# Outputs of an attention pair made beside the next pair's scores

## The chip, the cores and the metric

The kernel runs on one core of one Trainium2 chip, in one launch. The metric is the time of an execution in microseconds (us), as the median of three executions. The core has a matmul engine (TensorE, PE in the profile, with its weight loads listed apart as PEld), VectorE (DVE), ScalarE (ACT), GpSimd (POOL) and SyncE (SP), which issues nearly all transfers.

## The reference

There are 4 sequences of 768 tokens with 8 heads of 48. A gated linear attention comes first, then two feed-forward layers on 3072 tokens of 384 features with 2048 hidden ones, the first with a squared ReLU, the second with SiLU.

```python
for t in range(S):
    state = alpha[:, :, t, :, None] * state + np.einsum('bhd,bhe->bhde', k[:, :, t], v[:, :, t])
    y[:, :, t] = np.einsum('bhd,bhde->bhe', q[:, :, t], state)
x = y as (tokens, 384)
x = relu(x @ w_in) ** 2 @ w_out
g = x @ w2_in;  out = (g / (1 + exp(-g))) @ w2_out
```

## The kernel before

The 768 positions are six units of 128, and a unit holds those positions of all four sequences, 512 tokens. The attention of a unit is done in four pairs of heads, so there are 24 pairs n = 0 to 23 (PAIRS = 4). The first feed-forward layer of unit u runs in 16 steps, F = 16u to 16u + 15, one for each block of 128 hidden features. In step F TensorE makes `first_product` F (nine 128x512 matmuls, L1132: each product is a sum of three, of high and low parts of the operands), then `second_product` F - 2 (nine more, L1146). ScalarE makes three passes on the result of the first (`step` and `square_g`: L1429, L1432, L1435), VectorE one (`low_g`, L1810). The two banks `h_ps` take the first products in turn, by the parity of F; `z_ps` holds the second products' sums.

The attention of pairs 4 to 23 is done beside these steps, while the unit before is in the feed-forward layer. `stage_step` is a table of numbers written out by hand: it says in which step each job of a pair is done, and `beside(F)` gives the jobs of step F. For pairs 9 to 23 the jobs are: A (decays: transpose and two rows of scans on VectorE, L1660, L1688, L1703) in step 4n - 20 or 4n - 21; KQ (keys and queries scaled by the decays, VectorE, L1721, L1735) in 4n - 19; S (scores, TensorE, 64 small matmuls, L1007 and L1018) and I (the state's increment, TensorE, 32 small matmuls, L1040) in 4n - 18; Y (outputs, 64 small matmuls, L1109 and L1117) in 4n - 16. Pair 8 has S and I in step 16, Y in step 17. On TensorE S and Y stand between the first and the second product of their step, I behind the second product. I call such a group of small matmuls between large ones a visit.

The small matmuls write three banks, `jobs`. Scores and turned keys of a pair lie in `job_ps[1]` and `job_ps[2]`; its outputs lie in `job_ps[2]` and `job_ps[0]`. So the scores of pair n wait until the outputs of pair n - 1 have been read:

```python
                if n > PAIRS:
                    wait(pe, y_copied, y_count(n))
```

The reading is done in two parts. ScalarE copies the within-half part into `y_sb` (`y_copy`, L1377), then VectorE adds the other part to it (`y_stage`, L1790) and raises `y_copied`. VectorE also masks the scores (`s_stage`, L1747), and ScalarE copies the turned keys (`kt_copy`, L1366) when they are masked. After `y_copied` SP moves the outputs into `x_raw` (L639) and loads the values of pair n + 2 (L593). Everything on every engine is in program order, with semaphores between the engines. After step 95 the second layer follows (L1175, L1211, L1231), with no attention in it.

Of the kernel before, what the change touches and what calls it, by code (L numbers as in the profile page):

```python
# [6 lines left out]
ALU = mybir.AluOpType  # L7
ACT = mybir.ActivationFunctionType


BATCH, HEADS, SEQ, HD = 4, 8, 768, 48
# [6 lines left out]
UT = BATCH * P  # L18
PAIRS = HEADS // 2
ROWS = 64 + HD  # L20
# [5 lines left out]
HALF = P // 2  # L26
# [125 lines left out]
    return 256 * units if units < UNITS else 256 * (units - 1) + LAST_OUT  # L152


def stage_step(kind, n):

    if n < 2 * PAIRS:
        return {"A": 1, "KQ": 2 if n == PAIRS else 3, "S": 4, "I": 4, "Y": 5}[kind] + 3 * (n - PAIRS)
    if n == 2 * PAIRS:
        return {"A": 13, "KQ": 14, "S": 16, "I": 16, "Y": 17}[kind]  # L160
    return {"A": -20 if n == 2 * PAIRS + 1 else -21, "KQ": -19, "S": -18, "I": -18, "Y": -16}[kind] + 4 * n
# [36 lines left out]
def y_count(n):  # L198

    return min(n, MOVED) if n < PAIRS else n - PAIRS + MOVED  # L200
# [7 lines left out]
def beside(step):  # L208

    jobs = BESIDE.get(step, []) if isinstance(step, int) and step >= 0 else []  # L210
    return sorted(jobs, key=lambda j: ("S", "I", "A", "Y", "KQ").index(j[0]))


def repack_pieces(place):
# [24 lines left out]
def wait(eng, sem, value):  # L239
    if isinstance(value, int) and value <= 0:  # L240
        return
    eng.wait_ge(sem, value)
# [14 lines left out]
def build(nc, q, k, v, alpha, w1_in, w1_out, w2_in, w2_out, out):  # L257
    z_dram = nc.dram_tensor("z_scratch", (UNITS, DM, UT), F32, kind="Internal").ap()
    ctx = ExitStack()
    with ctx:  # L260
# [18 lines left out]
        with ExitStack() as one:  # L279
# [6 lines left out]
            y_sb = [sb(f"y_sb{i}", [ROWS, UT], F32, one) for i in range(2)]  # L286
# [134 lines left out]
        h_ps = [bank(f"h_ps{i}") for i in range(2)]  # L421
        z_ps = [bank(f"z_ps{i}") for i in range(KD)]

        jobs = ctx.enter_context(nc.psum_tensor("jobs", [P, 3 * 512], F32))
        s_ps, y_ps = jobs[:, 0:1024], jobs[:, 512:1536]
        job_ps = [jobs[:, 1024:1536], jobs[:, 0:512], jobs[:, 512:1024]]
# [13 lines left out]
        def v_tile(n):  # L440
            return v_wide[n - MOVED][:, :, 0::2, :] if MOVED <= n < PAIRS else v_sb[n % 2][:]
# [10 lines left out]

        first_y, middle_y, later_y = z_ps[1], z_ps[0], (job_ps[2], job_ps[0])
        half_i = (job_ps[2], job_ps[1])

        half_score = [x[:].rearrange("s b t -> s (b t)")[:, 0:BATCH * HALF] for x in score]
# [12 lines left out]
        kt_copied, y_copied = sem("kt_copied"), sem("y_copied")  # L471
# [470 lines left out]
        def _(pe):  # L942
# [37 lines left out]
            def s_stage(n):  # L980

                wait(pe, k_scaled, n + 1)
                wait(pe, q_scaled, n + 1)

                wait(pe, s_copied, 2 * min(n, PAIRS - 1))
                if n > PAIRS:
                    wait(pe, y_copied, y_count(n))
                if n > PAIRS and has_state(n - 1):
                    wait(pe, state_made, n - PAIRS)
                if n >= PAIRS:  # L990
                    s_halves(n)
                    return
                for b in range(BATCH):
                    for h in (0, 1):
                        r = head_rows(h)
                        last = nc.tensor.matmul(job_ps[1 + h][:, tile(b)], kp[n % 2][r, tile(b)], qp[n % 2][r, tile(b)],
                                                start=True, stop=True)
                last.then_inc(s_made, 1)
# [93 lines left out]
            def y_halves(n):  # L1092

                wait(pe, decayed, n - PAIRS + 1)

                wait(pe, i_copied, PAIRS)
                v_flat = v_tile(n).rearrange("t b h d -> t (b h d)")  # L1100

                def to(bank, b, place):
                    rows = slice(0, 64) if b < 2 else head_rows(1)
                    return later_y[bank][rows, place * HALF:(place + 1) * HALF], 64 if b < 2 else HD
                for half in (0, 1):
                    for b in (0, 2, 1, 3):
                        for h in (0, 1):
                            out_cols, cols = to(h, b, 2 * (b % 2) + half)
                            nc.tensor.matmul(out_cols, half_state[half][head_rows(h), b * HD:b * HD + cols],  # L1109
                                             qp[n % 2][head_rows(h), b * P + half * HALF:b * P + (half + 1) * HALF],  # L1110
                                             start=True, stop=True, skip_group_check=True)
                for h in (0, 1):
                    for b in (0, 2, 1, 3):
                        for half in (0, 1):
                            tokens, at = slice(half * HALF, (half + 1) * HALF), (2 * b + h) * HD
                            out_cols, cols = to(half, b, BATCH + 2 * h + b % 2)
                            last = nc.tensor.matmul(out_cols, v_flat[tokens, at:at + cols],  # L1117
                                                    half_score[h][tokens, b * HALF:(b + 1) * HALF],
                                                    start=True, stop=True, skip_group_check=True)
                last.then_inc(y_made, 1)  # L1120
# [5 lines left out]
            def first_product(u, par, f, w_hi, w_lo, tiles=TILES):  # L1126
                wait(pe, act_made, NF * u + f - 1)
                for kk in tiles:
                    if f == 0:
                        wait(pe, x_lo_made, KD * u + TILES.index(kk) + 1)  # L1130
                    for n, (w, x) in enumerate(((w_hi, x_hi), (w_hi, x_lo), (w_lo, x_hi))):
                        last = nc.tensor.matmul(h_ps[f % 2][:], w[:, f, tile(kk)], x[par][:, kk, :],  # L1132
                                                start=(kk == TILES[0] and n == 0), stop=(kk == TILES[-1] and n == 2))
                if tiles[-1] == TILES[-1]:
                    last.then_inc(h_made, 1)
# [111 lines left out]
            for F in range(STEPS):  # L1247
                u, f = divmod(F, NF)
                if u == 0:
                    wait(pe, w_lo_made, 2 * f + 1)  # L1250
                first_product(u, u % 2, f, win_hi, win_lo, TILES[-1:] if F < 2 else TILES)
                if F == 0:
                    i_stage(PAIRS - 1)
                for kind, n in beside(F):
                    if not behind(kind, n):
                        stage(kind, n)
                if F == LAST_U + 4:
                    pe.wait_ge(held_made, 2)
                    pe.wait_ge(y_copied, y_count(LASTP + 1))
                    nc.tensor.matmul(job_ps[0][0:1, 0:1], all_held[:], ones[:], start=True, stop=True).then_inc(held_summed, 1)  # L1260
                if F >= LAG:
                    u, f = divmod(F - LAG, NF)
                    if u == 0:
                        wait(pe, w_lo_made, 2 * f + 2)
                    second_product(u, f, g_pair(F - LAG), wout_hi, wout_lo, u, 0)
                for kind, n in beside(F):
                    if behind(kind, n):
                        stage(kind, n)
# [69 lines left out]
        def _(act):  # L1338
# [31 lines left out]
            def y_copy(n):  # L1370
                y_slot_free(n // PAIRS, n % PAIRS)
                wait(act, y_made, n + 1)
                if n < PAIRS:
                    nc.scalar.activation(y_sb[n % 2][:], first_y[0:ROWS, :], ACT.Copy).then_inc(y_copied, 1)
                    return

                nc.scalar.activation(y_sb[n % 2][:].rearrange("p (c k t) -> p k c t", c=BATCH, k=2),  # L1377
                                     y_ps[0:ROWS, :].rearrange("p (k x) -> p k x", k=2)[:, :, UT // 2:].rearrange(
                                         "p k (c t) -> p k c t", c=BATCH), ACT.Copy).then_inc(within_copied, 1)
# [276 lines left out]
        def _(dve):  # L1656
# [129 lines left out]
            def y_stage(n):  # L1786

                wait(dve, within_copied, n - PAIRS + 1)
                sums = y_sb[n % 2][:].rearrange("p (h x) -> p h x", h=2)
                nc.vector.tensor_tensor(sums, y_ps[0:ROWS, :].rearrange("p (h x) -> p h x", h=2)[:, :, 0:UT // 2], sums,  # L1790
                                        ALU.add).then_inc(y_copied, 1)
# [94 lines left out]
            for F in range(STEPS):  # L1886
                u, f = divmod(F, NF)
                jobs_here = beside(F)
                for kind, n in jobs_here:
                    if kind == "S":  # L1890
                        s_stage(n)
                    if kind == "KQ":
                        k_stage(n)
                        if n != 2 * PAIRS:
                            q_turn(n)
                            q_stage(n)
# [21 lines left out]
                        a_scan(n)  # L1918
                        a_grow(n)
                for kind, n in jobs_here:  # L1920
                    if kind == "Y" and n != 2 * PAIRS - 1:
                        y_stage(n)
                if F in T_STEP:
                    low_t(T_STEP[F])
# [142 lines left out]
```

## Time and profile before

| | |
|---|---|
| median of 3 runs | 881.98 us (881.14 to 882.66) |
| the profiled execution's own time | 877.95 us |
| its span | 876.3 us |
| PE busy | 862.5 us |
| DVE busy | 541.2 us |
| ACT busy | 437.0 us |
| POOL busy | 104.2 us |
| TensorE clock granted | 1.00 over the span |

The span is the part of an execution that the profile covers. The own time is that of the same execution as the runs' times measure it. Busy times count each engine's own instructions, so an engine that is busy nearly all the span is likely to set it.

### The profile page before, as it was taken

The page shows a single profiled execution, that of the slowest core. Times are in us where ns is not written, and L with a number is a line of the kernel's source. Part 1 is how long each engine was busy: PE and PEld are TensorE (multiplying, and loading weights), DVE is VectorE, ACT ScalarE, POOL GpSimd, SP SyncE. Part 2 cuts the span into 40 slices and gives each one's busy share as a digit, 9 for nine tenths or more (in the row PEclk, how much of TensorE's full clock was granted, in tenths as well). Part 3 has the DMA queues.
Part 4 walks back from the last instruction along what each step waited for, and adds up shares of the span by engine and source line. Part 5 has one row for each costly group of instructions (what it writes and reads, how often), then busy time and mean ns, then how long its engine had stood idle before and what let it go on. Part 6 is the DMA issues. An engine that isn't in the chain of part 4 may idle for free.

```text
span 876.3 us, 17615 instructions
## 1 busy us (share of the span) xinstructions
PE 862.5 (98%) x6834; PEld 707.5 (81%) x6834; DVE 541.2 (62%) x1072; ACT 437.0 (50%) x770; POOL 104.2 (12%) x127
## 2 busy tenths in 40 slices
PE   6999989999999999999999999999999999999998
PEld 6777768788878788788888888888888888888898
DVE  7788876777767667664334556556754446766620
ACT  5765544455446445544666744445434436554510
POOL 3453300000000000000354003003030003000000
PEclk9999999999999999999999999999999999999999
DMA  8885434333333332300412352000130000110010
GB/s 171 229 236 126 99 67 120 74 76 103 71 81 87 102 79 67 103 20 13 149 43 71 61 113 78 0 1 1 46 100 0 1 1 1 36 37 1 1 48 28
DMA packets 134203, 60.03 MB, mean 69 GB/s; under 512 B 81824, under 2 KB 129312, under 8 KB 134112
## 3 DMA queue, kind: packets, MB, share of 16 engines
q1 hardware_dynamic: 130800, 58.14, 26.9%
q8 instruction: 56, 0.92, 0.4%
q10 hardware_dynamic: 3312, 0.69, 0.4%
q14 instruction: 35, 0.29, 0.1%
HBM read 45.02 MB, written 9.44 MB: 62 GB/s over the span
## 4 chain that ended last, share of the span: by engine, by line
PE 93%; DVE 4%; issue 1%; ACT 1%; DMA 0%; DVEq 0%; ACTq 0%
PE z_ps L1146 21%; PE h_ps L1132 21%; PE h_ps L1175 20%; PE z_ps L1211 11%; PE jobs L1211 7%; PE jobs L1231 3%; PE jobs L1007 1%; PE jobs L1040 1%; PE jobs L1109 1%; DVE decay L1703 1%; PE jobs L1018 1%; PE jobs L1117 1%; PE h_ps L1231 1%; DVE decay L1688 1%; PE z_ps L1078 0%
## 5 line engine op out<-in xcount | busy, mean ns | idle before, releaser
L1429 ACT ACTIVATE g<-h_ps 128x512 f32<-128x512 f32 x96 | 57.4, 598 | 177.5 <-PE h_ps L1132 175.4
L1523 ACT ACTIVATE sum<-sum 128x512 f32<-128x512 f32 x96 | 60.6, 631 | 137.2 <-DVE sum L1871 111.9
L1810 DVE TENSOR_TENSOR g_lo<-g,g_hi 128x512 fp32r<-128x512 f32 x96 | 67.6, 705 | 85.4 <-ACT g L1435 85.3
L1871 DVE TENSOR_TENSOR sum<-h_ps,sum 128x512 f32<-128x512 f32 x120 | 83.0, 691 | 57.1 <-PE h_ps L1175 54.4
L1132 PE MATMUL h_ps<-x_hi,win_hi 128*128 128x512 f32 x288 | 115.0, 399 | 1.2 <-ACT g L1429 0.8
L1146 PE MATMUL z_ps<-g_hi,wout_hi 128*128 128x512 f32 x282 | 114.4, 406 | 0.0
L1132 PE MATMUL h_ps<-x_hi,win_lo 128*128 128x512 f32 x288 | 112.4, 390 | 0.0
L1132 PE MATMUL h_ps<-x_lo,win_hi 128*128 128x512 f32 x288 | 112.2, 389 | 0.0
L1146 PE MATMUL z_ps<-g_hi,wout_lo 128*128 128x512 f32 x282 | 110.2, 391 | 0.0
L1146 PE MATMUL z_ps<-g_lo,wout_hi 128*128 128x512 f32 x282 | 110.1, 390 | 0.0
L1175 PE MATMUL h_ps<-s_hi,t_hi 128*128 128x512 f32 x264 | 103.0, 390 | 0.2 <-DVE sum L1871 0.2
L1175 PE MATMUL h_ps<-s_hi,t_lo 128*128 128x512 f32 x264 | 102.7, 389 | 0.0
L1175 PE MATMUL h_ps<-s_lo,t_hi 128*128 128x512 f32 x264 | 102.7, 389 | 0.0
L1866 DVE TENSOR_TENSOR ring_lo<-sum,ring_hi 128x512 fp32r<-128x512 f32 x80 | 58.2, 728 | 64.3 <-ACT ring_hi L1536 64.3
L1132 PEld LDWEIGHTS h_ps<-x_hi,win_hi 128*128 128x128 f32 x288 | 54.0, 188 | 13.8 <-POOL win_lo L835 1.2
L1132 PEld LDWEIGHTS h_ps<-x_hi,win_lo 128*128 128x128 f32 x288 | 54.0, 188 | 11.7
L1146 PEld LDWEIGHTS z_ps<-g_hi,wout_hi 128*128 128x128 f32 x282 | 52.9, 188 | 12.2
L1132 PEld LDWEIGHTS h_ps<-x_lo,win_hi 128*128 128x128 f32 x288 | 54.1, 188 | 10.5
L1432 ACT ACTIVATE g_hi<-g 128x512 fp32r<-128x512 f32 x96 | 60.7, 632 | 3.1
L1146 PEld LDWEIGHTS z_ps<-g_hi,wout_lo 128*128 128x128 f32 x282 | 52.9, 188 | 11.5
L1146 PEld LDWEIGHTS z_ps<-g_lo,wout_hi 128*128 128x128 f32 x282 | 53.0, 188 | 10.0
L1435 ACT ACTIVATE g<-g 128x512 f32<-128x512 f32 x96 | 59.3, 617 | 0.0
(169 smaller groups left out, 1532.8 us busy)
## 6 DMA issues: line engine op xcount, KB each, us to landing
z_scratch<-z_sb SPq DMA_DIRECT2D x18, 256.0 KB, 2.7
pre<-z_scratch SPq DMA_DIRECT2D x18, 256.0 KB, 3.9
v_sb<-in_v SPq DMA_DIRECT2D x44, 96.0 KB, 2.6
out_x<-z_stage SPq DMA_DIRECT2D x80, 48.0 KB, 1.7
nat_a<-in_alpha SPq DMA_DIRECT2D x40, 88.0 KB, 2.3
nat_k<-in_k SPq DMA_DIRECT2D x40, 88.0 KB, 2.4
nat_q<-in_q SPq DMA_DIRECT2D x40, 88.0 KB, 2.2
nat_a<-in_alpha SPq DMA_DIRECT2D x40, 80.0 KB, 2.8
```

Source lines behind the costliest of these rows:

```text
L1132: last = nc.tensor.matmul(h_ps[f % 2][:], w[:, f, tile(kk)], x[par][:, kk, :], start=(kk == TILES[0] and n == 0), stop=(kk == TILES[-1] an ...
L1146: last = nc.tensor.matmul(z_ps[m][:], w[:, f, tile(m)], x, start=(f == 0 and n == 0), stop=(f == NF - 1 and n == 2), skip_group_check=True)
L1175: last = nc.tensor.matmul(bank[:], w[j][:, tile(t)], y[:, x, :], start=(c == 0 and k == 0), stop=(c == len(FACTORS[r]) - 1 and k == 2))
L1211: last = nc.tensor.matmul(pair_bank(t, m), w[f][:, tile(m)], x, start=(first and c == 0), stop=(final and c == 2), skip_group_check=True)
L1231: last = nc.tensor.matmul(token_ps[b][:, 0:DM], x[:, tile(b)], w[f][:], start=(f == 0 and n == 0), stop=(f == NF - 1 and n == 2))
L1429: nc.scalar.activation(g[f % 2][:], h_ps[f % 2][:], ACT.Relu).then_inc(act_made, 1)
L1432: nc.scalar.activation(high, g[f % 2][:], ACT.Copy if second else ACT.Square).then_inc(g_hi_made, 1)
L1435: nc.scalar.activation(g[f % 2][:], g[f % 2][:], ACT.Square).then_inc(g_made, 1)
L1523: nc.scalar.activation(at[:], at[:], ACT.Silu).then_inc(silu_made, 1)
L1810: nc.vector.tensor_tensor(low, g[f % 2][:], high.bitcast(F32), ALU.subtract).then_inc(g_lo_made, 1)
L1866: nc.vector.tensor_tensor(low, s_b[TILE_IN[i]][:], high.bitcast(F32), ALU.subtract).then_inc(tile_lo_made, 1)
L1871: nc.vector.tensor_tensor(to[:], h_ps[(PRODUCTS * n + r) % 2][:], other[:], ALU.add).then_inc(summed, 1)
```

## The change

For the first three pairs of each attention unit from unit 2 on (n = 8, 9, 10, 12, 13, 14, 16, 17, 18, 20, 21, 22: twelve pairs, those for which `beside_scores(n)` holds), job Y moves from its own step to that of S of pair n + 1. That is step 18 for pair 8, and step 4n - 14 for the others, so one step later for pair 8 and two for the others. In the visit Y stands ahead of S. The last pair of each unit keeps its step. One of the two banks that the outputs use changes: in place of `job_ps[2]` it is the `h_ps` bank of the first product of the step before, which is also the bank that the first product of the next step will write. So Y waits for the first ScalarE pass on the old product, and the next first product waits for `y_copied` of this pair; the scores no longer wait for it. As the two banks no longer lie side by side, ScalarE's copy and VectorE's addition are each two instructions of half the size.

```diff
+def beside_scores(n):
+    return n >= 2 * PAIRS and n % PAIRS < PAIRS - 1
...
 def stage_step(kind, n):
+    if kind == "Y" and beside_scores(n):
+        return stage_step("S", n + 1)
...
-    return sorted(jobs, key=lambda j: ("S", "I", "A", "Y", "KQ").index(j[0]))
+    return sorted(jobs, key=lambda j: ("Y", "S", "I", "A", "KQ").index(j[0]))
...
-        first_y, middle_y, later_y = z_ps[1], z_ps[0], (job_ps[2], job_ps[0])
+        first_y, middle_y = z_ps[1], z_ps[0]
+        def later_y(n):
+            return (h_ps[(stage_step("Y", n) - 1) % 2][:] if beside_scores(n) else job_ps[2], job_ps[0])
...
# TensorE, s_stage
-                if n > PAIRS:
+                if n > PAIRS and not beside_scores(n - 1):
                     wait(pe, y_copied, y_count(n))
# TensorE, y_halves
+                if n > PAIRS:
+                    wait(pe, y_copied, y_count(n))
+                if beside_scores(n):
+                    wait(pe, act_made, stage_step("Y", n))
# TensorE, ahead of first_product(F)
+                for kind, n in beside(F - 1):
+                    if kind == "Y" and beside_scores(n):
+                        pe.wait_ge(y_copied, y_count(n + 1))
# ScalarE, y_copy
+                if beside_scores(n):
+                    to = y_sb[n % 2][:].rearrange("p (c k t) -> p k c t", c=BATCH, k=2)
+                    for k in (0, 1):
+                        last = nc.scalar.activation(to[:, k], later_y(n)[k][0:ROWS, UT // 2:]..., ACT.Copy)
+                    last.then_inc(within_copied, 1)
+                    return
# VectorE, y_stage
+                if beside_scores(n):
+                    for k in (0, 1):
+                        to = y_sb[n % 2][:, k * UT // 2:(k + 1) * UT // 2]
+                        last = nc.vector.tensor_tensor(to, later_y(n)[k][0:ROWS, 0:UT // 2], to, ALU.add)
+                    last.then_inc(y_copied, 1)
+                    return
# VectorE, the loop over F: such a y_stage stands right behind s_stage and ahead of k_stage and low_g
```

TensorE's order from the first product of step 17 to the second product of step 18, before. The rows of L1109 and L1117 are Y of pair 8, those of L1007 and L1018 are S of pair 9; a row that only repeats is left out at each "...".

```order
L1132 MATMUL h_ps<-x_hi,win_lo 128x512
L1109 MATMUL jobs<-qp,score 64x64 x2
...
L1117 MATMUL jobs<-score,v_sb 48x64 x2
L1146 MATMUL z_ps<-g_hi,wout_hi 128x512
...
L1132 MATMUL h_ps<-x_hi,win_lo 128x512
L1007 MATMUL jobs<-qp,kp 64x64 x16
L1018 MATMUL jobs<-ident,kp 64x48 x16
L1146 MATMUL z_ps<-g_hi,wout_hi 128x512
```

The same stretch of TensorE's order in the changed kernel, where the lines are L1147 for the first product, L1161 for the second, L1124 and L1132 for Y and L1018 and L1029 for S.

```order
L1147 MATMUL h_ps<-x_hi,win_lo 128x512
L1161 MATMUL z_ps<-g_hi,wout_hi 128x512
...
L1147 MATMUL h_ps<-x_hi,win_lo 128x512
L1124 MATMUL h_ps<-qp,score 64x64
L1124 MATMUL jobs<-qp,score 64x64
...
L1132 MATMUL h_ps<-score,v_sb 48x64
L1132 MATMUL jobs<-score,v_sb 48x64
L1018 MATMUL jobs<-qp,kp 64x64 x16
L1029 MATMUL jobs<-ident,kp 64x48 x16
L1161 MATMUL z_ps<-g_hi,wout_hi 128x512
```

The large matmuls of step 17 now follow each other, and Y stands in the visit of S, with its banks taken in turn from `h_ps` and `jobs`.

VectorE's order over the same steps before, from the scaling of pair 9's queries in step 17 to the decay of the state in step 18.

```order
L1735 TENSOR_TENSOR qp<-w_ring,decay 112x512
L1810 TENSOR_TENSOR g_lo<-g,g_hi 128x512
L1790 TENSOR_TENSOR y_sb<-jobs,y_sb 112x512
L1747 TENSOR_TENSOR score<-jobs,causal 128x256 x2
L1810 TENSOR_TENSOR g_lo<-g,g_hi 128x512
L1772 TENSOR_TENSOR score<-state,decay 112x192
```

And the same stretch of VectorE in the changed kernel.

```order
L1760 TENSOR_TENSOR qp<-w_ring,decay 112x512
L1841 TENSOR_TENSOR g_lo<-g,g_hi 128x512
L1772 TENSOR_TENSOR score<-jobs,causal 128x256 x2
L1817 TENSOR_TENSOR y_sb<-h_ps,y_sb 112x256
L1817 TENSOR_TENSOR y_sb<-jobs,y_sb 112x256
L1841 TENSOR_TENSOR g_lo<-g,g_hi 128x512
L1797 TENSOR_TENSOR score<-state,decay 112x192
```

The addition of the outputs has moved from ahead of the masking of the next pair's scores to behind it, in two halves.

## Rows read from the trace of the kernel before

**Rows 1.** The page: busy time by engine, and the chain that ended last.

```profile
PE 862.5 (98%) x6834; PEld 707.5 (81%) x6834; DVE 541.2 (62%) x1072; ACT 437.0 (50%) x770; POOL 104.2 (12%) x127
...
PE 93%; DVE 4%; issue 1%; ACT 1%; DMA 0%; DVEq 0%; ACTq 0%
```

**Rows 2.** Waits over the span: who waited for whom, us in total, times, longest.

```profile
DVE score L1747 <- PE jobs L1018: 38.0, 20, 2.5
...
PEld jobs L1109 <- issue: 7.1, 20, 0.4
...
PE jobs L1007 <- DVE y_sb L1790: 2.4, 1, 2.4
```

**Rows 3.** TensorE's timeline, steps 60 and 61: start us, us, engine, line, tiles.

```profile
331.78 0.39 PE L1132 MATMUL h_ps<-x_hi,win_lo 128*128 128x512 f32 x1
332.10 0.68 PE L1109 MATMUL jobs<-qp,score 48*64 48x64 f32 x32
332.59 0.65 PE L1117 MATMUL jobs<-score,v_sb 64*48 64x64 f32 x32
333.17 0.50 PE L1146 MATMUL z_ps<-g_hi,wout_hi 128*128 128x512 f32 x1
...
335.35 0.39 PE L1132 MATMUL h_ps<-x_hi,win_hi 128*128 128x512 f32 x1
...
337.39 0.39 PE L1146 MATMUL z_ps<-g_hi,wout_hi 128*128 128x512 f32 x1
...
339.43 0.39 PE L1132 MATMUL h_ps<-x_hi,win_hi 128*128 128x512 f32 x1
```

**Rows 4.** TensorE's timeline, pair 19's scores in step 58, pair 20's in step 62.

```profile
321.79 0.69 PE L1007 MATMUL jobs<-qp,kp 48*64 48x64 f32 x32
322.30 0.63 PE L1018 MATMUL jobs<-ident,kp 48*64 48x48 f32 x32
...
325.74 0.50 PE L1132 MATMUL h_ps<-x_hi,win_hi 128*128 128x512 f32 x1
...
341.56 0.69 PE L1007 MATMUL jobs<-qp,kp 48*64 48x64 f32 x32
```

**Rows 5.** ScalarE's and VectorE's timelines, step 58.

```profile
323.06 0.62 ACT L1435 ACTIVATE g<-g 128x512 f32<-128x512 f32 x1
...
323.17 0.76 DVE L1747 TENSOR_TENSOR score<-jobs,causal 128x256 f32<-128x256 f32 x2 [2.03 <-PE jobs L1018]
323.85 0.68 DVE L1810 TENSOR_TENSOR g_lo<-g,g_hi 128x512 fp32r<-128x512 f32 x1
```

**Rows 6.** Groups of instructions, by line: busy us, mean ns, idle before.

```profile
L1747 DVE TENSOR_TENSOR score<-jobs,causal 128x256 f32<-128x256 f32 x40 | 15.1, 420 | 38.0 <-PE jobs L1018 38.0
...
L1790 DVE TENSOR_TENSOR y_sb<-jobs,y_sb 112x512 f32<-112x512 f32 x20 | 13.7, 686 | 0.0
...
L1377 ACT ACTIVATE y_sb<-jobs 112x512 f32<-112x512 f32 x20 | 11.6, 579 | 0.0
```

**Rows 7.** TensorE's and VectorE's timelines, steps 17 and 18.

```profile
121.24 0.39 PE L1132 MATMUL h_ps<-x_hi,win_lo 128*128 128x512 f32 x1
124.06 0.69 PE L1007 MATMUL jobs<-qp,kp 48*64 48x64 f32 x32 [2.43 <-DVE y_sb L1790]
124.55 0.66 PE L1018 MATMUL jobs<-ident,kp 48*64 48x48 f32 x32
...
121.91 0.69 DVE L1735 TENSOR_TENSOR qp<-w_ring,decay 112x512 f32<-112x512 f32 x1
...
123.12 0.68 DVE L1790 TENSOR_TENSOR y_sb<-jobs,y_sb 112x512 f32<-112x512 f32 x1
```

**Rows 8.** SP's timeline, steps 57 to 60: transfers issued.

```profile
317.10 3.68 SPq L639 DMA_DIRECT2D x_raw<-y_sb  x6
320.90 1.05 SPq L593 DMA_DIRECT2D v_sb<-in_v  x2
...
331.66 1.75 SPq L608 DMA_DIRECT2D nat_a<-in_alpha  x4
```

More of the change, by code:

```diff
@@ L1103, in to @@
                     rows = slice(0, 64) if b < 2 else head_rows(1)
-                    return later_y[bank][rows, place * HALF:(place + 1) * HALF], 64 if b < 2 else HD
+                    return later_y(n)[bank][rows, place * HALF:(place + 1) * HALF], 64 if b < 2 else HD
                 for half in (0, 1):
@@ L1374, in y_copy @@
                     nc.scalar.activation(y_sb[n % 2][:], first_y[0:ROWS, :], ACT.Copy).then_inc(y_copied, 1)
+                    return
+                if beside_scores(n):
+                    to = y_sb[n % 2][:].rearrange("p (c k t) -> p k c t", c=BATCH, k=2)
+                    for k in (0, 1):
+                        last = nc.scalar.activation(to[:, k], later_y(n)[k][0:ROWS, UT // 2:].rearrange("p (c t) -> p c t", c=BATCH),
+                                                    ACT.Copy)
+                    last.then_inc(within_copied, 1)
                     return
@@ L1891, in _ @@
                         s_stage(n)
+                for kind, n in jobs_here:
+                    if kind == "Y" and beside_scores(n):
+                        y_stage(n)
+                for kind, n in jobs_here:
                     if kind == "KQ":
@@ L1920, in _ @@
                 for kind, n in jobs_here:
-                    if kind == "Y" and n != 2 * PAIRS - 1:
+                    if kind == "Y" and n != 2 * PAIRS - 1 and not beside_scores(n):
                         y_stage(n)
```

## The prediction

> **What bounds the kernel now.** I read the page first, for which engine is full and which makes up the chain that ended last. TensorE is busy 98% of the span and is 93% of the chain, VectorE 62% busy and 4% of the chain [rows 1]. So a change counts by what it does to TensorE's stretch of work, by its idle time or by the time of its instructions. I read the waits next. In steps 0 to 95 TensorE hardly waits for anybody; one wait stands out, 2.4 us of the scores (L1007) for the addition of the outputs (L1790), and it occurs once [rows 2]. The same view has a second kind of row: the weight loads of L1109 show 7.1 us of idle time before them in 20 visits, 0.355 us each, put down to issue, so every visit pays something to begin. Then I read TensorE's timeline over one step with a visit and one without, which gives what a visit costs.
>
> A clean group of nine large matmuls takes 339.43 - 337.39 = 2.04 us, 0.227 us for one [rows 3]. In step 60 the last large matmul before Y starts at 331.78 and the first product of the next step at 335.35, 3.57 us later. Without the visit it would be ten matmuls, 2.27 us. The visit costs 1.30 us. Its first 32 small matmuls last 0.49 us, start to start (332.10 to 332.59), with no change to large ones in it. If the second 32 take the same, the small work is 0.98 us, and the remaining 0.32 us is paid for going in and out: 0.32 in place of 0.23 us from the last large start to the first small one, about 0.09 us at the end of the second 32, and a slow pair of large matmuls behind it (the nine from 333.17 to 335.35 take 2.18, not 2.04 us).
>
> **Merging the visits.** The number of matmuls stays, 64 for Y and 64 for S, with the same sizes; they are only put together. Of the two passages in and out one is left. Is there a price where Y goes over to S? The trace has no such place. The nearest are the seams within a visit: L1109 to L1117 changes both the tile (48*64 to 64*48) and the operands and costs nothing that I can see (0.49 us for the 32), and L1007 to L1018 is at 0.51 us [rows 3, 4]. Bounds: nothing, or the whole 0.32 us again, so that merging brings nothing. I take nothing, since both seams are nearer to it than any passage from 128*128 tiles. A longer run of small matmuls could be limited by how fast they are issued, but in step 18 the scores began after a long wait, with nothing queued ahead, and still took 0.49 us for their 32 (124.06 to 124.55) [rows 7].
> So 0.32 us for each of eleven merged visits: **3.5 us**. The twelfth, in step 18, is different.
>
> **Step 18.** Here the scores of pair 9 could have followed the product at 121.24 + 0.32 = 121.56 and started at 124.06, 2.50 us late, because VectorE's addition of pair 8's outputs ended at 123.12 + 0.68 = 123.80 [rows 7]. From that end to TensorE's start are 0.26 us. What is late next if that wait goes? The scores also need pair 9's queries, scaled by VectorE until 121.91 + 0.69 = 122.60. VectorE's run of work up to there has no gap since the masks of pair 8 in step 16, which the change does not touch, so this end stays at 122.60, and the scores start at 122.60 + 0.26 = 122.86. That is 1.20 us earlier than before. Pair 8's outputs fill part of the gap: with no visit in step 17 the product of step 18 starts its last matmul at 121.24 - 1.30 = 119.94, Y takes from 120.26 to about 121.24 and TensorE is idle from there to 122.86. The bounds of this term are nothing (another wait of equal length takes its place) and the whole 2.50 us. I take **1.2 us**, since both ends of it are rows.
>
> **The new wait.** The first product of step F + 1 now waits for `y_copied` of the pair whose outputs were made in step F, and everything of TensorE is queued behind it. I work it out for step 58, where S and I of pair 19 stand, with Y of pair 18 put ahead. All of S moves by 0.98 us. VectorE's masks began at 323.17 and so begin at 324.15; the two of them last 0.76 us, and what follows begins 0.08 us before their end (323.17 + 0.76 against 323.85) [rows 5], at 324.83. The additions are two of 112x256. No such addition is in the trace; the nearest is the mask, 128x256, also read from these banks, at 420 ns each, 0.76 us for two [rows 6]. They end at 325.59. The upper bound is two at the full size's 686 ns, which with the same overlap is about 0.6 us later, 326.2. With the 0.26 us of [rows 7] TensorE may go on at 325.85 (326.45 by the upper bound). The product is due at 325.74 + 0.98 = 326.72 [rows 4]. So 0.87 us of slack, 0.27 us by the upper bound: the cost is **nothing**, and the cover is the second product and the state's visit of the same step. ScalarE's part is earlier: its third pass starts at 323.06 and ends at 323.68 [rows 5], the outputs are made at about 321.79 + 0.98 = 322.77, and two copies at no more than the 579 ns of the whole [rows 6] end by 324.9, as the masks do. The wait of Y for the first ScalarE pass of the step before is free: that product ended two groups of nine, 4.08 us, before Y, and the pass follows it at once.
>
> The Trainium skill, page Perfetto Trace Analysis, section Optimizing Tensor Performance, says that independent groups of matmuls should rotate through different banks, so that the reading of one overlaps the matmuls of the next. The change does the opposite for one bank of twelve pairs, and by that advice alone the next first product would stand still; the rows above say that other groups, into other banks, cover the reading. What it would mean here is the third rival below. Its section Optimizing Scalar/DVE Operations gives about 125 ns (VectorE) and 51 ns (ScalarE) of access overhead for an instruction on PSUM. By that the split would add, as an estimate, 0.18 us to the reading, against the 0.87 us of slack, and the sum would stay.
>
> **The rest.** VectorE gets twelve more instructions and ScalarE twelve. VectorE stood idle 38.0 us in 20 visits before the masks, 1.9 us each [rows 2], so a little more work is absorbed. The masks, the copy of turned keys and the state's visit all come later by the same 0.98 us as the scores. On SP the move to `x_raw` (3.68 us of issuing) and the load of values (1.05 us) go behind one more set of key and query loads. The values of pair n + 2 are then issued about 9 us after the visit begins, about 10 us before their use in the visit of the pair after next, one period of 341.56 - 321.79 = 19.77 us [rows 4] later. The next decays' load at 331.66 [rows 8] is still after them: 325.59 + 3.68 + 1.05 = 330.3. No cost.
>
> **The sum.** 3.5 + 1.2 = 4.7 us off. The profiled execution's own 877.95 us (span 876.3, so 1.65 us lie around it) becomes 873.2. It is 4.03 us under the runs' median, and I take the difference off that: 881.98 - 4.7 = **877.3 us**.
>
> **The rivals.**
> *The wait in step 18 only changes its name.* For it: VectorE is continuously busy there. Against it: the chain to 122.60 is read from rows. Then 3.5 us remain, 878.5 us. Chance 0.08.
> *Merging saves nothing.* A passage is paid for a change between jobs, not for a change of matmul size, or the added wait ahead of the product costs a new start of the weight loads, at most the 0.355 us of [rows 2], which cancels the 0.32. For it: no row shows Y against S. Against it: the seams within a visit. Then 1.2 us remain, 880.8 us, no measurable change. Chance 0.12.
> *The bank shared with the product stalls it.* This is the side on which it gets slower. `y_copied` would come later than I work out, in each of the twelve. Its price begins at 0.87 us of lateness, and it decides the sign once the stall is above 4.7 / 12 = 0.39 us, so at 1.26 us of lateness. With a stall of 1 us each it is 881.98 - 4.7 + 12 = 889.3 us. For it: the slack is under a microsecond, and the pass through two engines is long. Against it: even full-sized additions fit. Chance 0.07.
> The forecast itself has 0.73.
>
> **How the numbers follow.** The likeliest case spans 876.0 (3.5 + 2.5 off) to 878.5. The range adds the runs' own scatter below, and above it reaches toward the case in which merging saves nothing: 875.8 to 880.6. It leaves out that case at its full size and the slower one. A measurement of this kernel can tell about 0.2%, 1.8 us, from no change. Faster by more than this: 0.73 + 0.08 = 0.81; within it: 0.12; slower: 0.07.
>
> **What would show it.** In the changed kernel's timeline a merged visit should last about 1.96 us of small work and one passage; the period from one such visit to the next about 19.45 us where it was 19.77. In step 18 the scores should be released by the scaled queries, some 1.2 us earlier, and no first product after a merged visit should wait for the addition. I am wrong if waits of the first product for the addition appear about twelve times, or if the place between Y and S shows the idle time of a visit's start.

## The result and the profile after

The changed kernel takes 873.87 us (median of 6 runs, 872.94 to 875.04); the kernel before, in 6 runs, 881.35 us (878.11 to 882.66). The ratio is 0.9926 with a 95% interval of 0.9908 to 0.9945, so the change takes off about 6.5 us (4.8 to 8.1). I had forecast 4.7 us off and 877.3 us, in a range from 875.8: right in direction, too small in size, and the measured time lies below the range.

The page of the changed kernel, busy time by engine and the chain that ended last:

```profile
span 872.9 us, 17660 instructions
PE 858.8 (98%) x6834; PEld 708.2 (81%) x6834; DVE 542.2 (62%) x1084; ACT 435.6 (50%) x782; POOL 104.2 (12%) x127
...
PE 94%; DVE 3%; issue 1%; ACT 1%; DMA 0%; ACTq 0%; DVEq 0%
```

Against [rows 1] the number of matmuls is the same, and TensorE is busy 3.7 us less, although none was taken out: each matmul is busy until its end, which overlaps the next one's start, so the slower starts on the way into and out of a visit count as busy time too, and there are fewer of them. Next the merged visit in step 58, TensorE from the last large matmul ahead of it:

```profile
316.62 0.39 PE L1147 MATMUL h_ps<-x_hi,win_lo 128*128 128x512 f32 x1
316.94 0.27 PE L1124 MATMUL h_ps<-qp,score 48*64 48x64 f32 x1
...
317.90 0.68 PE L1018 MATMUL jobs<-qp,kp 48*64 48x64 f32 x32
318.39 0.65 PE L1029 MATMUL jobs<-ident,kp 48*64 48x48 f32 x32
318.97 0.50 PE L1161 MATMUL z_ps<-g_hi,wout_hi 128*128 128x512 f32 x1
...
321.86 0.50 PE L1147 MATMUL h_ps<-x_hi,win_hi 128*128 128x512 f32 x1
```

Y takes 317.90 - 316.94 = 0.96 us and S follows with no gap; from 316.62 to 318.97 are 2.35 us, with only one passage in and out. From the scores of one merged visit to those of the next are 317.90 - 298.47 = 19.43 us (19.45 forecast). In this kernel L1398 is ScalarE's copy and L1817 VectorE's addition. VectorE and ScalarE in the same step:

```profile
319.26 0.75 DVE L1772 TENSOR_TENSOR score<-jobs,causal 128x256 f32<-128x256 f32 x2 [2.26 <-PE jobs L1029]
319.93 0.41 DVE L1817 TENSOR_TENSOR y_sb<-h_ps,y_sb 112x256 f32<-112x256 f32 x1
320.26 0.41 DVE L1817 TENSOR_TENSOR y_sb<-jobs,y_sb 112x256 f32<-112x256 f32 x1
...
318.73 0.36 ACT L1398 ACTIVATE y_sb<-h_ps 112x256 f32<-112x256 f32 x1
318.99 0.38 ACT L1398 ACTIVATE y_sb<-jobs 112x256 f32<-112x256 f32 x1
```

The additions end at 320.67 and the product starts at 321.86, 1.19 us later; less the 0.26 us of [rows 7] the slack is 0.93 us (0.87 forecast). No wait of the first product for the addition is in the view of waits. And step 18, VectorE's scaled queries and TensorE's scores:

```profile
122.11 0.69 DVE L1760 TENSOR_TENSOR qp<-w_ring,decay 112x512 f32<-112x512 f32 x1
...
122.91 0.69 PE L1018 MATMUL jobs<-qp,kp 48*64 48x64 f32 x32 [1.32 <-issue]
```

The scores start at 122.91 (122.86 forecast) where they started at 124.06 [rows 7], and an idle time of 1.32 us is left where it was 2.43. The row names no releaser ("issue"), but the scores wait for the scaled queries, and these end at 122.11 + 0.69 = 122.80, 0.11 us before. That is less than the 0.26 us of the forecast; on the other hand this whole trace stands 0.2 us later (its first large matmul starts at 27.59, before at 27.40).

From the start of its first large matmul to the start of its very last one, a small one (873.08 before, 868.05 after), TensorE takes 845.68 us before and 840.46 us after, 5.22 us less. I call this TensorE's stretch. The large matmuls of the two traces side by side put 1.3 us of it in steps 17 and 18 and 0.35 us in each of the eleven other merged visits. The spans differ by only 3.4 us, because the start of this profiled execution was 0.2 us longer and its end 1.6 us (4.5 us from the last matmul's end, against 2.9). The medians differ by 7.5 us, while the ratio, which isn't that of the medians, stands for 6.5 us. So neither the difference of the spans nor that of the medians is the 5.2 us of the traces, and the experiments had to say where the rest is.

### The profile page after: what moved, and what is told of

It is laid out like the page before. It is cut to its first block, busy times and chain, and to the rows that moved or that the text cites. A ratio compares the mean times of both kernels' runs of the same rounds, so it can differ in the third digit from the quotient of the medians.

```text
span 872.9 us, 17660 instructions
## 1 busy us (share of the span) xinstructions
PE 858.8 (98%) x6834; PEld 708.2 (81%) x6834; DVE 542.2 (62%) x1084; ACT 435.6 (50%) x782; POOL 104.2 (12%) x127
## 4 chain that ended last, share of the span: by engine, by line
PE 94%; DVE 3%; issue 1%; ACT 1%; DMA 0%; ACTq 0%; DVEq 0%
PE h_ps L1147 21%; PE z_ps L1161 21%; PE h_ps L1190 21%; PE z_ps L1226 11%; PE jobs L1226 7%; PE jobs L1246 3%; PE jobs L1051 1%; PE jobs L1018 1%; PE jobs L1029 1%; PE h_ps L1246 1%; DVE decay L1728 1%; PE h_ps L1124 1%; PE jobs L1124 1%; PE jobs L1132 1%; PE h_ps L1132 0%
## 5 line engine op out<-in xcount | busy, mean ns | idle before, releaser
L1147 PE MATMUL h_ps<-x_hi,win_hi 128*128 128x512 f32 x288 | 115.0, 399 | 1.2 <-ACT g L1454 0.8
L1161 PE MATMUL z_ps<-g_hi,wout_hi 128*128 128x512 f32 x282 | 113.1, 401 | 0.0
L1147 PE MATMUL h_ps<-x_hi,win_lo 128*128 128x512 f32 x288 | 112.4, 390 | 0.0
L1147 PE MATMUL h_ps<-x_lo,win_hi 128*128 128x512 f32 x288 | 112.2, 390 | 0.0
L1161 PE MATMUL z_ps<-g_lo,wout_hi 128*128 128x512 f32 x282 | 110.1, 390 | 0.0
L1161 PE MATMUL z_ps<-g_hi,wout_lo 128*128 128x512 f32 x282 | 110.0, 390 | 0.0
L1147 PEld LDWEIGHTS h_ps<-x_hi,win_hi 128*128 128x128 f32 x288 | 54.0, 188 | 13.9 <-POOL win_lo L846 1.2
L1147 PEld LDWEIGHTS h_ps<-x_hi,win_lo 128*128 128x128 f32 x288 | 54.0, 188 | 11.6
L1147 PEld LDWEIGHTS h_ps<-x_lo,win_hi 128*128 128x128 f32 x288 | 54.1, 188 | 10.4
L1161 PEld LDWEIGHTS z_ps<-g_hi,wout_hi 128*128 128x128 f32 x282 | 52.9, 188 | 11.9
L1161 PEld LDWEIGHTS z_ps<-g_hi,wout_lo 128*128 128x128 f32 x282 | 52.9, 188 | 11.4
L1161 PEld LDWEIGHTS z_ps<-g_lo,wout_hi 128*128 128x128 f32 x282 | 53.0, 188 | 10.2
```

The source lines that it names most:

```text
L1161: last = nc.tensor.matmul(z_ps[m][:], w[:, f, tile(m)], x, start=(f == 0 and n == 0), stop=(f == NF - 1 and n == 2), skip_group_check=True)
```

## The experiments

In all, twelve runs, each against the kernel before on the same chip. The theories: A, the rest is scatter at the ends; B, the executions of the kernel before lose time in the middle that its one profile did not show; C, what is lost there is TensorE's clock, behind the idle time of step 18; D, it is something else of the old order. The shortest span is over all executions of a kernel's timing; the clock is the mean granted in each. A mean of 0.999 does not show a drop in the middle: in the changed kernel's profile, at 0.999, the clock is 1.00 past the last matmul and 0.50 only in the last 1 us of the span. So the table counts 0.998 or less.

| kernel | median us | ratio (95%) | shortest span | executions with clock 0.998 or less |
|---|---|---|---|---|
| before_again | 879.8 | 0.9993 (0.9979 to 1.0008) | 876.2 | 7 of 12 |
| only_18 | 877.44 | 0.9963 (0.9948 to 0.9978) | 874.8 | 0 of 8 |
| without_18 | 876.73 | 0.9949 (0.993 to 0.9968) | 872.3 | 5 of 6 |
| unit1_too | 872.64 | 0.9908 (0.9892 to 0.9924) | 870.5 | 0 of 6 |
| add_behind_g | 874.84 | 0.9938 (0.9914 to 0.9962) | 871.1 | 0 of 4 |
| add_behind_state | 903.94 | 1.027 (1.0239 to 1.03) | 900.3 | 4 of 4 |
| gap_shorter | 880.3 | 0.9988 (0.9976 to 1.0001) | 875.5 | 9 of 12 |
| gap_longer | 875.84 | 0.9946 (0.993 to 0.9962) | 872.9 | 5 of 6 |
| y_apart | 878.5 | 0.9969 (0.9956 to 0.9983) | 874.8 | 0 of 6 |
| s9_later | 872.38 | 0.9902 (0.9886 to 0.9917) | 870.6 | 0 of 4 |
| changed_again | 874.05 | 0.992 (0.9903 to 0.9937) | 871.1 | 0 of 6 |
| s9_again | 871.05 | 0.9892 (0.9875 to 0.991) | 869.1 | 0 of 5 |

**The kernel before again.** No edit.

> The kernel before, unchanged, against itself, to see how its executions scatter. In the two traces TensorE's large matmuls stand 5.03 us earlier at the end of the attention and the same 5.03 us earlier at the last one, and the start is 0.18 us later: 5.2 us. The medians differ by 7.5 us. Theory A: what is above 5.2 us is scatter that both kernels have, at the ends of an execution (after the last matmul the kernel before had 2.9 us left, the changed one 4.5 us in its profile but 2.6 in other executions). Then the executions here have spans from 876.3 to about 878.5 and the ratio is 1.000. Theory B: in most executions of the kernel before TensorE stalls somewhere in the middle, which the profiled one did not show; then spans of 879 to 881 are frequent, and a profile of such an execution has a stall in steps 0 to 95 that is not in the first one.

Theory B. TensorE in step 18 of this profile:

```profile
123.94 0.78 PE L1007 MATMUL jobs<-qp,kp 48*64 48x64 f32 x32 [2.42 <-DVE y_sb L1790]
124.43 1.12 PE L1018 MATMUL jobs<-ident,kp 48*64 48x48 f32 x32
125.47 0.79 PE L1146 MATMUL z_ps<-g_hi,wout_hi 128*128 128x512 f32 x1
126.07 0.63 PE L1146 MATMUL z_ps<-g_lo,wout_hi 128*128 128x512 f32 x1
126.49 0.63 PE L1146 MATMUL z_ps<-g_hi,wout_lo 128*128 128x512 f32 x1
```

The wait is that of [rows 7], but behind it large matmuls follow each other at 0.43 us in place of 0.227. The stretches around it (busy times, then the granted clock, as a share of full speed):

```profile
110.00:121.00 11.00, 11.00 (x195) 8.85 (x192) 9.57 (x29) 6.62 (x12) 0.00 (x0) 1.00 0.26 59
121.00:124.00 3.00, 0.58 (x7) 0.18 (x6) 2.65 (x4) 2.31 (x5) 0.00 (x0) 1.00 0.00 0
124.00:128.00 4.00, 4.00 (x70) 3.42 (x71) 1.62 (x4) 0.49 (x1) 0.00 (x0) 0.57 0.28 71
128.00:140.00 12.00, 12.00 (x141) 9.53 (x140) 7.25 (x24) 4.61 (x8) 0.00 (x0) 1.00 0.62 164
```

After 2.4 us without work TensorE ran on the lower level, 1.2 GHz, for most of 4 us, and then on 2.4 GHz again. Its stretch took 847.21 us against 845.68 in the first profile: 1.53 us for the lower clock. The profile that I had read was one of the few without it. In the 55 executions of the kernel before that the twelve runs were compared with, the mean clock was 1.000 in 7 and 0.998 to 0.994 in 48; in before_again's own 12 it was 0.998 or less in only 7.

**Step 18 alone, and all but step 18.** `beside_scores` is changed.

```diff
-    return n >= 2 * PAIRS and n % PAIRS < PAIRS - 1
+    return n == 2 * PAIRS                                # only_18
+    return n > 2 * PAIRS and n % PAIRS < PAIRS - 1       # without_18
```

> Only pair 8 is made beside the next scores (step 18), the eleven others keep their visit. Read from the trace this step gave 1.3 us (forecast 1.2), so about 1.3 us less than the kernel before, ratio 0.9985. By theory B, if what the odd executions lose is in this step (VectorE is continuously busy there), it is 3 us or more, ratio below 0.9965.

> The eleven other pairs are made beside the next scores, pair 8 is not. Each merged visit gave 0.35 us in the trace, so 3.9 us less than the kernel before, ratio 0.9956; the wait of 2.4 us in step 18 is there again. If merging saved nothing it would be 1.000; if the rest of the 7.5 us hangs on the merged visits, 0.993.

The shortest spans (876.2 us is that of before_again) give the parts as the traces have them: 876.2 - 874.8 = 1.4 us for step 18, 876.2 - 872.3 = 3.9 us for the eleven others, 5.3 us together as in the changed kernel's 870.9. The ratios give step 18 a different size: 0.9963 is 3.3 us (1.9 to 4.6), and 0.9949 for the others is 4.5 us (2.8 to 6.2). The executions of without_18 still have the lower clock (0.998 or 0.996 in five of six), and its profile, at 0.996, has it behind a wait of 2.44 us, through all of this stretch:

```profile
124.00:130.00 6.00, 5.82 (x73) 4.63 (x73) 1.62 (x4) 0.49 (x1) 0.00 (x0) 0.50 0.42 94
```

Here the lower level lasted about twice as long as in before_again, and it cost twice as much: the stretch is 844.82 us, 3.0 us over the 845.68 - 3.9 = 841.8 due without it. The executions of only_18 don't have the lower clock. So most of what is over the traces' 5.2 us goes with step 18.

**A shorter wait in the kernel before, a longer one in the changed kernel.**

```diff
# gap_shorter, kernel before, VectorE, ahead of low_g
+                if F == stage_step("Y", 2 * PAIRS):
+                    y_stage(2 * PAIRS)
# gap_longer, changed kernel; TensorE, s_stage
+                if n == 2 * PAIRS + 1:
+                    pe.wait_ge(g_lo_made, NF + 2)
# VectorE, low_g, step 17 computed twice
+                if isinstance(F, int) and F == NF + 1:
+                    nc.vector.tensor_tensor(low, g[f % 2][:], high.bitcast(F32), ALU.subtract).then_inc(extra, 1)
+                    dve.wait_ge(extra, 1)
```

> The kernel before with one instruction of VectorE moved: pair 8's addition ahead of the low part of g in step 17, so that TensorE's wait in step 18 is 0.6 us shorter, about 1.85 us in place of 2.43, with nothing merged. In the runs so far an execution of a kernel with the wait of 2.4 us mostly has a mean granted clock of 0.998 or 0.996 and a span 1.4 to 3 us above that kernel's shortest, and one without it never under 0.999. Theory C: the idle time lets the granted clock fall to 1.2 GHz behind it; then, if 1.85 us is too short for that, the clocks are 1.000 or 0.999, the shortest span is 875.6 (0.6 under 876.2), and the ratio about 0.997. If the clock still falls as before, the ratio is 0.9993, only the 0.6 us. Theory D: what falls is due to something else of the old order (the masks, the banks): then too the clock is as before.

> The changed kernel, with the scores of pair 9 in step 18 also waiting for the low part of g of step 17, which VectorE computes twice: some 1.3 us more than the 1.32 us of idle time, 2.6 us in all, everything else as in the change. Theory C: the granted clock falls again behind this idle time in most executions (0.998 or 0.996), so the shortest span is about 872.2 (870.9 + 1.3) and the median about 2 us above that, ratio 0.9965. Theory D (it is not the idle time): clocks of 1.000 and 0.999 as in the changed kernel, ratio 0.994.

TensorE's scores in the two profiles, gap_shorter and then gap_longer:

```profile
123.56 0.73 PE L1007 MATMUL jobs<-qp,kp 48*64 48x64 f32 x32 [1.81 <-DVE y_sb L1790]
```

```profile
124.15 0.69 PE L1021 MATMUL jobs<-qp,kp 48*64 48x64 f32 x32 [2.70 <-DVE g_lo L1847]
```

And a stretch behind them, in gap_longer:

```profile
124.10:130.00 5.90, 5.85 (x106) 4.70 (x107) 2.46 (x7) 0.49 (x1) 0.00 (x0) 0.71 0.54 182
130.00:140.00 10.00, 10.00 (x45) 8.26 (x44) 6.83 (x23) 3.89 (x7) 0.00 (x0) 1.00 0.29 64
```

My hope that 1.8 us would be short enough failed: the clock fell in 9 of 12 executions, and only the 0.6 us showed, in the shortest span (875.5 to 876.2) as in the ratio (0.9988). But gap_longer decides between C and D. It has the merged visits, the new banks and the new order, and only the idle time is back, 2.70 us; the lower clock came back with it, in 5 of 6 executions. TensorE's stretch is 843.34 us against 840.46, which is 2.9 us for 1.38 us more of idle time. That is theory C. The ratio does not say so: it is 0.9946 (0.993 to 0.9962), which leaves out the 0.9965 that I gave for C and holds the 0.994 that I gave for D. But the 0.9965 does not fit the spans that I expected by C: a median about 2 us above 872.2 is a span of 874.2 us, which is a ratio near 0.994 too, and the measured median span is 874.25. So the ratio can't tell the two theories apart; the clocks and the stretch do. Over all kernels here whose idle time in step 18 is 1.4 us or less, 45 executions with those of the changed kernel, no mean clock was under 0.999.

The Trainium skill, page TensorE: Matmul & The Clock Gate, Part 1, says that the array's clock has two levels, 1.2 and 2.4 GHz, that the lower one is the default and that activity releases the upper. These traces agree on the two levels: 0.50 and 1.00 are the granted values of the stretches behind and before the idle time.

**Where the 0.35 us of a merged visit come from.** In y_apart Y stands ahead of the first product of its new step and S behind it.

```diff
# TensorE, loop over F, ahead of first_product(F)
+                for kind, n in beside(F):
+                    if kind == "Y" and beside_scores(n):
+                        stage(kind, n)
```

> The changed kernel with Y ahead of the first product of the step and S behind it: the same step, banks, waits and copies, but two visits in place of one. If the gain of 0.35 us a pair is the passage between large and small matmuls, the eleven give it back: shortest span 870.9 + 3.9 = 874.8, ratio about 0.9965. If it is due to the move itself (fewer waits in the old step, other banks), it stays at 870.9. In step 18 Y before or behind the product changes nothing, the scores start when the queries are scaled; but the idle time there is then one piece of about 1.3 us as before.

The shortest span is 874.8 us, TensorE's stretch 844.43 us, 3.97 us longer than in the changed kernel (0.36 for each of eleven), and the clock stays up; the idle time of step 18 is 1.06 us there. So it is the passage between large and small matmuls that the change saves, and not the later step or the other banks.

**How much slack the new wait has.** In add_behind_g and add_behind_state the additions of merged pairs stand behind `low_g`, or behind the state's update.

```diff
# VectorE; the loop is moved from behind s_stage
                 if F > 0:
                     low_g(u, f, g_pair(F), False, NF * u)
+                for kind, n in jobs_here:
+                    if kind == "Y" and beside_scores(n):
+                        y_stage(n)                       # add_behind_g; in add_behind_state behind i_stage
```

> The change, but VectorE adds the outputs behind the low part of g (0.60 us later) in the merged steps. In the trace of the changed kernel the addition in step 58 ends at 320.67 and the product starts at 321.86; with 0.26 us from one to the other there are 0.93 us of slack, 0.33 us after this edit. So no change against the changed kernel, ratio 0.9926 to the kernel before. If the slack is really smaller than 0.6 us each of 12 visits stalls, and it is up to 3 us slower than the changed kernel.

> The change, but VectorE adds the outputs behind the state's update in the merged steps, which itself waits for TensorE's visit just ahead of the product. In step 58 the update ends at 323.16, the two additions 0.74 us later, TensorE may go on 0.26 us after that, at 324.2, where the product was due at 321.86: 2.3 us of stall in each of 12 visits, 27 us more than the changed kernel, about 901 us. It prices the rival in which the bank shared with the product stalls it. If the wait were hidden elsewhere it would stay at 874.

0.6 us more are free: TensorE's stretch is 840.50 us against 840.46. Behind the state's update the waits are there, twelve of them:

```profile
PE h_ps L1147 <- DVE y_sb L1817: 22.0, 12, 1.9
```

```profile
323.05 0.50 PE L1147 MATMUL h_ps<-x_hi,win_hi 128*128 128x512 f32 x1 [1.94 <-DVE y_sb L1817]
323.38 0.39 PE L1147 MATMUL h_ps<-x_lo,win_hi 128*128 128x512 f32 x1
...
324.26 0.63 PE L1147 MATMUL h_ps<-x_lo,win_hi 128*128 128x512 f32 x1
324.69 0.63 PE L1147 MATMUL h_ps<-x_hi,win_lo 128*128 128x512 f32 x1
```

The kernel takes 30 us more than the changed one for 22 to 24 us of waits (23.5 by the weight loads' rows); the large matmuls behind this one again go at 0.43 us, and the mean clock is 0.992 or 0.990. Of the twelve idle times in this one trace nine are 1.94 us and three 1.53 us. The clock fell behind three of the nine and behind one of the three; here stretches behind a longer one with and one without the fall, then behind a shorter one with it:

```profile
174.00:177.00 3.00, 3.00 (x9) 2.34 (x8) 0.00 (x0) 0.19 (x1) 0.00 (x0) 0.50 0.17 48
216.00:220.00 4.00, 4.00 (x18) 3.31 (x19) 0.00 (x0) 1.70 (x3) 0.00 (x0) 1.00 0.24 64
...
428.73 0.50 PE L1147 MATMUL h_ps<-x_hi,win_hi 128*128 128x512 f32 x1 [1.53 <-DVE y_sb L1817]
...
430.00:433.00 3.00, 3.00 (x9) 2.33 (x8) 0.00 (x0) 0.75 (x2) 0.00 (x0) 0.50 0.18 51
```

Four falls at 1.5 us are 6 us, which with 23.5 us of waits is the 29.5 us that the stretch is longer (869.97 to 840.46). So less than 1.8 us of idle time can be enough, and eight of the twelve had no such price. The rival in which the shared bank stalls the product is priced by this, and it would have been worse than I made it.

**Two steps further.** In unit1_too pairs 4 and 5 are merged too; s9_later also has pair 9's scores and state in step 19.

```diff
-    return n >= 2 * PAIRS and n % PAIRS < PAIRS - 1
+    return n >= 2 * PAIRS and n % PAIRS < PAIRS - 1 or n in (PAIRS, PAIRS + 1)   # unit1_too, s9_later
...
+    if n == 2 * PAIRS + 1 and kind in ("S", "I"):                                # s9_later, stage_step
+        return 19
```

> The change, with pairs 4 and 5 of unit 1 also made beside the next scores (steps 7 and 10). By 0.35 us for each merged visit 0.7 us less than the changed kernel, ratio 0.9918 to the kernel before, if VectorE, which has a pair every three steps there, is not late: then first products of steps 8 and 11 would wait for the addition, and it would be no faster.

> The change with pairs 4 and 5 merged too, and pair 9's scores and state in step 19 in place of 18, with pair 8's outputs. In step 18 TensorE still waited 1.3 us for the scaled queries; a step later they are long there. 1.3 us less than the kernel with pairs 4 and 5 merged: shortest span 869.2, ratio 0.989 to the kernel before. Against it: VectorE has the masks, the addition and the next decays in one step then, and pair 10's queries for step 22 may be late; then a wait of up to 1 us stands there.

> The changed kernel, unchanged, on the same chip as the next. From the last matmul's end to the end of the span the profiles of all kernels so far have either 2.8 to 2.9 us or 4.5 to 4.8 us (the last output transfer, issued by ScalarE, lands after 1.7 or 3.3 us). If that is scatter of its own, both lengths come again: spans of 870.9 and 872.8, no mean clock under 0.999, ratio about 0.993.

> The kernel with pairs 4 and 5 merged and pair 9's scores in step 19, again. Its last matmul ended 2.1 us earlier than that of the changed kernel, from the first product on, yet its four executions all had spans of 870.6 to 870.7, with the long end. If the long end is scatter, some spans of 868.8 come now and the median falls to 870.5 to 872; if this kernel always has it, the spans stay at 870.7 and the time at 872.4.

unit1_too is 0.3 us shorter in TensorE's stretch (840.15), under half of the 0.7 us expected. Its first pair brings 0.36 us, its second only 0.14, and there the scores start 0.23 us after the last matmuls of the outputs, not at once. Pair 6's queries were just scaled then, and end 0.11 us before, as in step 18:

```profile
76.22 0.86 DVE L1760 TENSOR_TENSOR qp<-w_ring,decay 112x512 f32<-112x512 f32 x1
...
77.19 0.69 PE L1018 MATMUL jobs<-qp,kp 48*64 48x64 f32 x32
```

So VectorE was late after all, for the scores and not for the product; where the stretch gives back the other 0.2 us is not shown. s9_later takes 838.37 us, 1.8 us less than unit1_too: the idle time of step 18 (1.33 us) is gone, and no wait of the scores stands in step 22. The other 0.45 us I did not take apart. Its first four executions all had the long end, and the gain did not show; in the second timing spans of 869.1 to 869.3 came up beside 870.2 and 870.3. Its 871.05 us, ratio 0.9892 (0.9875 to 0.991), is the fastest that I found.

The long end is in the changed kernel's first profile, the short one in that of before_again: the last output transfer, issued by ScalarE, by its KB and its time to landing in us.

```profile
out_x<-z_stage ACTq DMA_DIRECT2D x1, 96.0 KB, 3.3
```

```profile
out_x<-z_stage ACTq DMA_DIRECT2D x1, 96.0 KB, 1.7
```

Both lengths come in one and the same kernel: 3.6 us in the profile of s9_later, 1.7 in that of s9_again, and changed_again has three spans of 871.1 to 871.3 and three of 872.7 to 873.2. The kernel before with one instruction moved, gap_shorter, has 3.4 us. What makes it long stays open.

## Why the prediction was right or wrong

*What bounds the kernel*: right. TensorE's stretch of work shortened by what the change took from it, and everything behind it in program order kept the whole 5.2 us.

*Merging the visits, 0.32 us each, 3.5 us*: right in mechanism, slightly small. It is 0.35 us each and 3.9 us. That the seam from Y to S costs nothing is in the rows at 317.90, and y_apart shows that the passage is the cause.

*Step 18, 1.2 us*: this is the step that failed. The direct gain was 1.3 us. That the scores started within 0.05 us of the forecast is partly luck: the 0.11 us from the queries' end to the scores, taken as 0.26, and the later start of the whole trace nearly cancel. But the term counted the idle time alone. The price of TensorE's lower clock behind it was put at nothing without a word. In 48 of 55 executions of the kernel before the mean clock was at 0.998 or less, and the profiles that have it show it behind this idle time, at 1.5 us or, where it lasts twice as long, 3.0 us; behind the 1.3 us that the change leaves it was never seen. Measured, the term is 3.3 us (1.9 to 4.6, only_18).

*The sum*: here the same error entered a second time. Of the 8.1 us between the 881.98 us that I started from and the measured 873.87, 0.6 us is only that the first three runs of the kernel before were slower than the six of the result (881.35). I made the sum against the one profiled execution and took the 4.03 us between it and the median as an offset that stays. It was not: the profiled execution, with a clock of 1.000, was one of the few without the drop. Medians of spans show it: 879.2 us over the 55 executions before, 3.0 above the shortest (876.2, in before_again); 872.0 over the twelve after, 1.1 above the shortest (870.9). The difference, 7.2 us, is 5.3 us of work plus 1.9 us. I take the 1.9 us for the lower clock, since 48 of 55 at 1.5 to 3.0 us each are 1.3 to 2.6 us on average; but both medians also hold the short and the long ends, and before_again's own 12 have a median span of only 878.1 us, so its size is rough. That a few runs of 881 to 882 stood beside a profile of 878 was in my table, and I didn't ask what it was.

*The new wait costs nothing*: right, 0.93 us of slack for 0.87, and add_behind_g confirms that 0.6 us of it are free. The split of the reading, estimated at 0.18 us, cost about 0.12: the two copies take 0.06 us longer than the whole one, and so do the two additions. The advice on rotating banks (the Trainium skill, page Perfetto Trace Analysis, section Optimizing Tensor Performance) did not decide here, as other groups stood in between. *The rest*: right; no new waits.

*The rivals*: that step 18's wait only changes its name, that merging saves nothing, and that the bank stalls the product are all refuted, the last with its price.

## What to carry to other kernels

Ask of each wait on the bounding engine not only how long it is but how fast the engine runs after it: here 1.8 us and more of idle TensorE in step 18 mostly cost another 1.5 to 3 us in the next matmuls, and 1.3 us did not. It is no fixed limit: in add_behind_state eight of twelve idle times of 1.5 and 1.9 us cost nothing more than themselves. Compare the profiled execution's own time with the spread of the runs before making a sum against it; a profile well under the median may be without something that most runs have. And small matmuls between large ones were best put together, at 0.35 us a passage, as long as the bank they use is read while other groups run.

## What the runs showed of the hardware

- Behind idle times of 1.81, 2.42, 2.44 and 2.70 us in step 18 TensorE was at 1.2 GHz in the profiles of gap_shorter, before_again, without_18 and gap_longer; the first profile of the kernel before had 2.43 us and no drop, and by their mean clocks 7 of 55 of its executions were free of it. With 1.33 us or less it was never seen there. In add_behind_state it came behind three of nine idle times of 1.94 us and one of three of 1.53 us. Which escape, the profiles don't tell.
- The lower level cost 1.5 us where it lasted most of 4 us (before_again, gap_longer), and 3.0 us where it lasted from 124 to 130 us (without_18).
- The last 96 KB transfer took either 1.7 or 3.3 us and more to land (3.9 in changed_again).
- Halving a PSUM read cost little: two copies of 112x256 at 363 and 375 ns, started 0.26 us apart, take 0.64 us, and two additions at 412 ns, started 0.33 us apart, 0.74 us, against 579 and 686 ns for the whole ones [rows 6].
- From VectorE's end to TensorE's start were 0.26 us after the addition (before) and 0.11 us after the scaled queries (step 18 of the changed kernel, step 10 of unit1_too).
